# One Strassen level (seven quarter products) for the first product of the second layer

## What is computed

```python
h = x @ w_in            # x: 1536 tokens x 512, w_in: 512 x 2048
r = np.maximum(h, 0.0)
g = r * r
return g @ w_out        # w_out: 2048 x 512
```

## Time and profile before

| what | us |
|---|---|
| median of 3 runs | 483.92 (483.80 to 483.97) |
| span of the profiled execution, first to last instruction | 481.6 |
| around the span (median less span) | 2.3 |
| TensorE busy in the span | 471.1 |
| VectorE busy | 278.1 |
| ScalarE busy | 212.9 |
| GpSimd busy | 103.8 |

### The profile page before, as it was taken

The page is one execution under the profiler, slowest core; times in us unless marked ns, Lnnn a source line. Parts: engine busy times, 40 slices in busy tenths (PEclk is TensorE's granted clock), DMA queues, the critical chain, the costliest instruction groups (busy, mean ns, idle before and its releaser), DMA issues.

```text
span 481.6 us, 7337 instructions
## 1 busy us (share of the span) xinstructions
PE 471.1 (98%) x2634; PEld 382.5 (79%) x2634; DVE 278.1 (58%) x514; ACT 212.9 (44%) x559; POOL 103.8 (22%) x155
## 2 busy tenths in 40 slices
PE   7889999999999999999999999999999999999997
PEld 5667787887788888878888888888888888888885
DVE  3899889898989888767755354322222233222232
ACT  3677777656777666242324253222222232222221
POOL 2366323231321232739930000000000000000000
PEclk9999999999999999999999999999999999999999
DMA  7931437765569424498400000200000020000002
GB/s 214 315 92 50 136 85 215 205 192 159 149 180 219 113 57 120 119 252 240 90 1 0 1 0 1 87 0 0 0 0 0 0 87 1 0 0 1 0 1 87
DMA packets 51990, 41.80 MB, mean 87 GB/s; under 512 B 28088, under 2 KB 38072, under 8 KB 51448
## 3 DMA queue, kind: packets, MB, share of 16 engines
q1 hardware_dynamic: 51192, 40.74, 29.9%
q10 hardware_dynamic: 768, 0.66, 0.5%
HBM read 30.38 MB, written 11.01 MB: 86 GB/s over the span
## 4 chain that ended last, share of the span: by engine, by line
PE 91%; DVE 3%; POOL 2%; ACT 1%; DMA 1%; issue 1%; ACTq 0%; DVEq 0%; POOLq 0%
PE score_ps L1675 27%; PE h_ps L1689 14%; PE w_ps L1516 13%; PE h_ps L1476 12%; PE w_ps L1689 7%; PE wt_ps L1689 7%; PE o_ps L1438 4%; PE score_ps L1404 2%; PE wt_ps L1404 2%; PE wt_ps L1415 1%; DMA x2T<-qT 1%; PE o_ps L1459 1%; POOL pT_own L576 1%; PE w_ps L1541 1%; DVE prob L1095 1%
## 5 line engine op out<-in xcount | busy, mean ns | idle before, releaser
L1675 PE MATMUL score_ps<-x2T_hi,w2in_hi 128*128 (+1 forms) x192 | 74.8, 389 | 0.0
L1675 PE MATMUL score_ps<-x2T_hi,w2in_lo 128*128 (+1 forms) x192 | 74.7, 389 | 0.0
L1675 PE MATMUL score_ps<-x2T_lo,w2in_hi 128*128 (+1 forms) x192 | 74.7, 389 | 0.0
L1328 DVE TENSOR_TENSOR e<-e 128x512 f32<-128x512 f32 x24 | 17.9, 744 | 82.0 <-ACT e L968 82.0
L1328 DVE TENSOR_TENSOR sq<-relu 128x512 f32<-128x512 f32 x24 | 17.2, 717 | 77.0 <-ACT relu L968 77.0
L968 ACT ACTIVATE relu<-score_ps 128x512 f32<-128x512 f32 x24 | 14.3, 597 | 90.5 <-PE score_ps L1675 90.5
L968 ACT ACTIVATE e<-score_ps 128x512 f32<-128x512 f32 x24 | 14.4, 599 | 89.7 <-PE score_ps L1675 89.7
L1675 PEld LDWEIGHTS score_ps<-x2T_lo,w2in_hi 128*128 128x128 f32 x192 | 36.0, 188 | 7.5
L1675 PEld LDWEIGHTS score_ps<-x2T_hi,w2in_hi 128*128 128x128 f32 x192 | 36.1, 188 | 7.5
L1675 PEld LDWEIGHTS score_ps<-x2T_hi,w2in_lo 128*128 128x128 f32 x192 | 36.0, 188 | 7.4
L742 ACT ACTIVATE prob<-sm,nbias 128x132 f32<-128x132 f32 (+1 forms) x96 | 37.6, 393 | 4.1 <-DVE nbias L1019 3.4
(11 more groups left out here) (192 smaller groups left out, 1095.0 us busy)
## 6 DMA issues: line engine op xcount, KB each, us to landing
u_dram<-uT SPq DMA_DIRECT2D x18, 256.0 KB, 3.2
lnT_raw<-u_dram SPq DMA_DIRECT2D x36, 128.0 KB, 2.9
w2in<-w_in SPq DMA_DIRECT2D x4, 1024.0 KB, 5.3
w2out<-w_out SPq DMA_DIRECT2D x8, 512.0 KB, 9.9
V<-v SPq DMA_DIRECT2D x12, 256.0 KB, 3.2
x2T<-x_dram SPq DMA_DIRECT2D x12, 256.0 KB, 4.8
x_dram<-x SPq DMA_DIRECT2D x44, 64.0 KB, 2.2
k_raw<-kT SPq DMA_DIRECT2D x20, 132.0 KB, 2.9
```

Of the source, the lines that this page charges most:

```text
L1328: nc.vector.tensor_tensor(sq[f % 2], relu[f % 2], relu[f % 2], ALU.mult).then_inc(sq_ready, 1)
L1675: done = mm(h2_ps[f % 2], ws[:, c, fs], xs[:, c, bass.ts(blk, BLK)], start=(c == 0 and i == 0), stop=(c == MC - 1 and i == 2))
```

## The change

The first product of layer two is done as one Strassen level (the form with seven products and fifteen sums). x (512 features x 768 tokens) and a piece of `w_in` (512 features x 2 x 128 units) are each cut in 2 x 2 quarters; four sums of quarters are made on each side, seven products of quarters are taken, and their sums are the four tiles of h. The tokens go in two passes of 768, each with 8 steps of 256 hidden units (two groups of 128): 16 steps. Token halves are 384 wide, so a product is 2 chunks x 3 = 6 matmuls of 384 columns.

Per step, each pass anew: SP loads a piece of `w_in` (two DMAs of 256 KB in rows of 512 bytes) and of `w_out` (512 KB); GpSimd makes the four sums of weights (128x256 each) and the lo parts (128x512, 128x1024, 128x256); ScalarE rounds; VectorE makes five sums with one operand in PSUM (128x384), the gate (relu times itself) and its lo parts in three parts (384, 768, 384 wide) and the lo part of `w_out` (128x1024). The x combinations (seven, 128x768 each) of pass 0 are summed by GpSimd and split by VectorE and GpSimd; those of pass 1 by VectorE in steps 2 to 6.

The relevant constants and the TensorE order:

```diff
-BLK = BANK
+PASSES = 2
+TS = T // PASSES
+TH = TS // 2
+NJ = C2 // 2
+NI = PASSES * NJ
+PRODUCTS = ((A11, B11, 0, True), (S2, T2, 1, True), (A12, B21, 0, False), (S3, T3, 1, False),
+            (S1, T1, 0, True), (A22, T4, 1, False), (S4, B22, 0, False))
+UNITS = tuple((tile, r, q) for tile, r, qs in ((0, 0, (0, 1, 2)), (1, 1, (0, 1, 2)), (2, 1, (3, 4, 5)), (3, 0, (3, 4, 5)))
+              for q in qs)
...
+            def multiply(i, n):
+                wk, xk, bank, opens = PRODUCTS[n]
...
+                if n == 0 and i:
+                    pe.wait_ge(added, 5 * i)
+                elif n == 1 and i:
+                    pe.wait_ge(added, 5 * i - 1)
+                elif n == 2:
+                    pe.wait_ge(p1_copied, i + 1)
+                elif n == 3:
+                    pe.wait_ge(added, 5 * i + 1)
+                elif n == 4:
+                    pe.wait_ge(corner_ready, i + 1)
+                elif n == 5:
+                    pe.wait_ge(added, 5 * i + 2)
+                elif n == 6:
+                    pe.wait_ge(added, 5 * i + 3)
+                for c in range(2):
+                    for k in range(3):
+                        ws, xs = ((w2_hi, xc_hi), (w2_hi, xc_lo), (w2_lo, xc_hi))[k]
+                        done = mm(prod_ps[bank], ws[i % 2][:, wk, c, :], xs[s][xk][:, c, :], start=(opens and c == 0 and k == 0),
+                                  stop=(c == 1 and k == 2), skip_group_check=True)
...
+            multiply(0, 0)
+            multiply(0, 1)
             project(NT - 2, 0, 24)
-            hidden2(0, 1, 2, 3)
+            multiply(0, 2)
+            multiply(0, 3)
             transpose_ln(NT - 1)
-            hidden2(0, 1, 3, 4)
-            project(NT - 1, 0, 12).then_inc(wo_half_read, 1)
+            multiply(0, 4)
+            project(NT - 1, 0, 12)
+            multiply(0, 5)
             project(NT - 1, 12, 24)
-            with pe.Fori(0, NB - 1) as blk:
-                block_b(blk, True)
-            block_b(NB - 1, False)
+            multiply(0, 6)
+            for i in range(1, NI):
+                multiply(i, 0)
+                multiply(i, 1)
+                project2(i - 1, 0, 4)
+                multiply(i, 2)
+                multiply(i, 3)
+                project2(i - 1, 4, 8)
+                multiply(i, 4)
+                multiply(i, 5)
+                multiply(i, 6)
+                project2(i - 1, 8, 12)
+            project2(NI - 1, 0, 12)
```

`added` counts VectorE's sums, five a step: sum_2, sum_3, lower_right, lower_left, upper_right. VectorE's order in a step:

```diff
+            for i in range(1, NI):
+                sum_2(i)
+                split_g(i - 1, 2)
+                if i == NJ + 1:
+                    copy_y(0, (3, 5))
+                split_wy(i)
+                sum_3(i)
+                gate_corner(i)
+                lower_right(i)
+                split_g(i, 0)
+                lower_left(i)
+                gate_sum(i, 1)
+                if i == 2:
+                    sum_x(T1, 0, x_quarter(0, 1), x_quarter(0, 0))
+                    sum_x(T2, 1, x_quarter(1, 1), x_combination(1, T1))
+                elif i == 3:
+                    sum_x(T3, 2, x_quarter(1, 1), x_quarter(0, 1))
+                    split_x(1, B11)
+                elif i == 4:
+                    split_x(1, T2)
+                    split_x(1, B21)
+                elif i == 5:
+                    split_x(1, T3)
+                    split_x(1, T1)
+                    dve.wait_ge(xc_split[T2], 2)
+                    sum_x(T4, 3, x_quarter(1, 0), x_combination(1, T2))
+                elif i == 6:
+                    split_x(1, T4)
+                    split_x(1, B22)
+                elif i == NJ:
+                    copy_y(0, (1,))
+                upper_right(i)
+                split_g(i, 1)
+                gate_sum(i, 2)
```

GpSimd's list:

```diff
+                if t == NT - 3:
+                    sum_x(T1, 0, x_quarter(0, 1), x_quarter(0, 0))
+                    sum_x(T2, 1, x_quarter(1, 1), x_combination(0, T1))
+                    sum_x(T3, 1, x_quarter(1, 1), x_quarter(0, 1))
                 if t + 2 < NT and not alone(t + 2):
                     gather_sinks(t + 2)
...
-            for f in range(C2):
-                if f == 3:
-                    inverse_std(NT - 1)
-                    pool.wait_ge(ln_ready, 2 * NT)
-                fs = slice(f * P, (f + 1) * P)
...
+            pool.wait_ge(scored, PAIRS * NT)
+            sum_w2(0)
+            split_w2_first(0)
+            split_w2_sums(0)
+            split_w2_last(0)
+            split_x(B21)
+            split_x(T3)
+            inverse_std(NT - 1)
+            pool.wait_ge(xc_split[T2], 1)
+            sum_x(T4, 3, x_quarter(1, 0), x_combination(0, T2))
+            for i in range(1, NI):
+                sum_w2(i)
+                split_w2_first(i)
+                split_w2_sums(i)
+                split_w2_last(i)
```

ScalarE's list in a step:

```diff
+            for i in range(1, NI):
+                copy_p1(i)
+                round_g(i - 1, 2)
...
+                round_wy(i)
+                if i + 1 < NI:
+                    round_w2(i + 1)
+                corner(i)
+                round_g(i, 0)
+                if i + 1 < NI:
+                    round_w2_sums(i + 1)
...
+                round_g(i, 1)
```

In layer one two orders change. TensorE's last step does 8 of the 24 products of tile 9 ahead of hidden(11), and 16 behind it:

```diff
-                project(n - 2, 0, 24)
+                project(n - 2, 0, 8)
                 pe.wait_ge(u_ready, 2 * n)
                 hidden(n, 0, 24)
+                project(n - 2, 8, 24)
```

```diff
             square_x2(NT - 4)
             for part in range(len(LN_PARTS)):
                 split_lnT(NT - 3, part)
+            split_xT(NT - 1)
             normalize_hidden(NT - 2)
-            split_xT(NT - 1)
             square_u(NT - 2)
-            split_x2T(0)
-            square_x2(NT - 3)
+            split_x(0, B11)
+            split_x(0, T2)
             hidden_max(NT - 1, 0)
             hidden_max(NT - 1, 1)
             hidden_max_all(NT - 1)
...
+            sum_2(0)
+            square_x2(NT - 3)
             normalize_hidden(NT - 1)
+            split_x(0, T1)
+            split_x(0, T4)
+            split_x(0, B22)
             square_x2(NT - 2)
...
+            sum_3(0)
             for part in range(len(LN_PARTS)):
                 split_lnT(NT - 1, part)
```

More of the change, by code:

```diff
@@ L513, in _ @@
[L513 to L525, removed]
@@ L529, in side_loads @@
+            for i in range(2, NI):
+                load_wy(i)
+                if i + 1 < NI:
+                    load_w2(i + 1)
+                if i == NJ + 2:
+                    store_y(0)
+            store_y(1)
+            sp.wait_ge(y_stored, 16 * (PASSES * YT + 1))
         def side_loads(act):
@@ L956, in _, with copy_y @@
+            def copy_y(s, qs):
+                for q in qs:
+                    act.wait_ge(y_done, YT * s + q + 1)
+                    nc.scalar.copy(y[:, q, :], y_ps[q]).then_inc(y_copied_act, 1)
             for part in range(len(LN_PARTS)):
@@ L1368, in _ @@
+            split_g(NI - 1, 2)
+            copy_y(1, (1, 3, 5))
         @block.tensor
@@ L1660, in _ @@
             last_step()
-            def hidden2(blk, f, first=0, last=MC):
-                g = blk * C2 + f
-                if first == 0:
-                    pe.wait_ge(w2in_split, f + 1)
-                    if f == 0:
-                        pe.wait_ge(x2T_split, blk + 1)
-                    if f >= 2 or since(blk, 1):
-                        pe.wait_ge(relu_ready, g - 1)
-                fs = slice(f * P, (f + 1) * P)
-                for c in range(first, last):
-                    for i in range(3):
-                        ws, xs = ((w2in_hi, x2T_hi), (w2in_hi, x2T_lo), (w2in_lo, x2T_hi))[i]
-                        done = mm(h2_ps[f % 2], ws[:, c, fs], xs[:, c, bass.ts(blk, BLK)],
-                                  start=(c == 0 and i == 0), stop=(c == MC - 1 and i == 2))
-                if last == MC:
-                    done.then_inc(h2_done, 1)
@@ new lines, in project2 @@
+            def project2(i, first, last):
+                j, s = i % NJ, i // NJ
+                for n in range(first, last):
+                    tile, r, q = UNITS[n]
+                    if n == 0:
+                        pe.wait_ge(wy_split, i + 1)
+                    if n % QH3 == 0:
+                        pe.wait_ge(g_split, 3 * i + (1, 2, 2, 3)[tile])
+                    if i == 0 and n == 2 * QH3:
+                        pe.wait_ge(x2_squared, NT)
+                    if s and j == 0 and r == q // QH3:
+                        pe.wait_ge((y_copied_act, y_copied_dve)[q % 2], q // 2 + 1)
+                    rows = slice(q % QH3 * P, (q % QH3 + 1) * P)
+                    for k in range(3):
+                        gs, ws = ((g_hi, wy_hi), (g_hi, wy_lo), (g_lo, wy_hi))[k]
+                        done = mm(y_ps[q], gs[i % 2][:, tile, rows], ws[i % 2][:, r, :],
+                                  start=(j == 0 and r == q // QH3 and k == 0), stop=(j == NJ - 1 and r != q // QH3 and k == 2))
+                    if j == NJ - 1 and r != q // QH3:
+                        done.then_inc(y_done, 1)
```

(2 more changed lines are left out.)

466 lines of the change are left out of this document (291 added, 175 removed).

## The result

| what | before | after |
|---|---|---|
| median, us | 483.86 (482.77 to 483.97, 4 runs) | 496.51 (495.46 to 497.01, 4 runs) |
| ratio after/before, 95% interval | | 1.0265 (1.0247 to 1.0282) |
| profiled span | 481.6 | 494.4 |

Slower by 12.65 us; the forecast was 492.8, in a range of 473 to 497.

What follows compares the result with a forecast made beforehand. The prediction took the kernel to be bound by the columns TensorE streams. From 483.9 us it took off 14.1 for products and added 4.8 (hidden(10)), 5.1 (seam) and 13.1 (x pieces): 492.8 us, range 473 to 497.

Steps and rivals of the forecast that it cites:

- products: Layer two's first product: 672 matmuls of 384 columns at 0.173 us replace 576 of 512, saving 14.1 us.
- hidden(10) late: Layer one: GpSimd's three x sums take turns with VectorE's normalizing and x split, delaying hidden(10) by 4.8 us.
- seam, waits: Where the layers meet: waits before project(10), project(11) and step 1's first product, +5.1 us, bounds 0.5 and 5.5.
- x pieces, steps 2 to 6: VectorE's x pieces, ahead of upper_right, take turns with GpSimd's weight sums and delay the next step's first product: +13.1 us.
- rival 4: Layer two's first product: weight load surfaces at 384 columns, 0.214 us each, 27 us more, near 520; chance 0.03.
- A steady step: New loop, step without x pieces: 15.44 us; more than 15.5 us would show the prediction wrong.
- P6's cover of 0.2 us: Each step's last of seven products: the lower_right sum is ready at 11.45 us, product due at 11.67, so no wait.
- rival 3: The 0.2 us cover of each step's seventh product fails too, 0.3 us in 15 steps: 497.3 us; chance 0.1.
- the second product keeps 576 matmuls of 512 columns: Layer two's second product: matmul number and width unchanged, priced at the old 0.227 us each, so no change in time.
- Each microsecond in which it waits is lost: TensorE throughout: bound by columns streamed, so a wait was priced at its own length, with no clock cost added.
- 1 and 2: First: all covers hold, 471.9 us, chance 0.2. Second: only the x pieces are free, 481.3 us, chance 0.14.
- rival 1: Covers hold: GpSimd's instructions fall between VectorE's; x sums, seam and x pieces cost bare time: 471.9 us; chance 0.2.

Runs made afterwards that it cites:

- upper_first: Kernel after, with VectorE in steps 2 to 6 doing upper_right, split_g and the last gate_sum before the x pieces: 484.58 us, ratio 1.0017.
- filled_wait: Kernel after, with 15 matmuls of no use put into TensorE's wait before hidden(10): 493.15 us, ratio 1.0198.
- ln_first: Kernel after, with VectorE doing tile 10's square, sum_3(0) and tile 11's split before the T4 and B22 splits: 493.41 us, ratio 1.0181.
- three_orders: Kernel after, with x pieces behind upper_right, GpSimd's x sums behind tile 10's x split, tile 11's split before T4 and B22's: 476.04 us, ratio 0.9838.

## Why the prediction was right, and what it had wrong

The sign held, and so did the place and the cause ("GpSimd and VectorE taking turns at one port") of each loss that was forecast. Two costs of another kind were not in the sum. The terms, in us, predicted and as the trace of after shows them:

| term | predicted | measured | from |
|---|---|---|---|
| products | -14.1 | -13.7 | 0.1733 apart, but 0.175 in P2 to P6 of even steps |
| hidden(10) late | +4.8 | +4.3 | 20.58 against 16.24 from hidden(9) |
| slow clock behind it | 0 | +2.9 | 8.33 against 5.44 |
| seam, waits | +5.1 | +3.5 | 0.4 + 2.4 + 1.0, less 0.3 there before |
| slow clock behind it | 0 | +1.6 | 4.26 + 1.39 against 2.99 + 1.06 |
| x pieces, steps 2 to 6 | +13.1 | +11.1 | 10.6 of waits less step 1's 0.7, and 5 x 0.24 |
| slow clock behind step 5 | 0 | +1.3 | 3.49 against 2.16 |
| pace of the second product | 0 | +2.6 | 2.79 and 2.75 for 12 against 2.72 |
| sum | +8.9 | +13.6 | spans: 494.4 - 481.6 = +12.8, and 0.8 that the trace of after was ahead |

The 0.24 is what a wait costs beside its length at full clock: the listed idle time begins with a matmul's result, 0.16 us after its slot, and the 12 matmuls behind a wait take some 0.08 more.

- **Products.** Right: 384 columns come every 0.1733 us, the columns and the same 0.0133, but for the 0.4 us of the even steps. The weight load did not surface (rival 4).
- **A steady step.** Said 15.44, measured 15.6 to 15.8. By the prediction's own sign ("if a step without pieces takes more than 15.5 us") this part is wrong. P6's cover of 0.2 us held in all 15 steps, so rival 3 (497.3) falls, though its total lies nearest. The step that failed is "the second product keeps 576 matmuls of 512 columns", taken at the old price: it kept the number and not the pace.
- **Steps 2 to 6.** "In turns" is what the timeline shows, instruction by instruction. The forecast's P0 at 17.7 us into the step came at 17.5 to 17.6, and 19.3 with three pieces at 19.0. The term is smaller than 13.1 for this and because the steady step was longer to begin with. `upper_first` shows the price: 11.9 us, waits and clock together, with its own new 0.5 taken off.
- **hidden(10).** GpSimd's sums took 1.88 and 1.98 us, said 1.85; the wait ended 1.2 us earlier than I had it, of which 0.8 is the start of the trace.
- **The seam.** project(11) waited 2.13, said 3.0, P0 of step 1 0.74, said 0.75. project(10) had 1.7 and took 0.4: the chain behind hidden_exp was drawn too late. That term was oversized.
- **The step that is missing.** "Each microsecond in which it waits is lost" was too kind: in the trace of after a wait of 3.57, of 2.13 and of 3.05 us was each followed by matmuls at half pace, 5.8 us in all. I read "the granted clock is full in every slice" as a fact about the kernel and not as one about its gaps: before, TensorE's longest was the 1.7 us at the start of the kernel, and every later one at most 0.93. `filled_wait` shows it for hidden(10), where the wait is filled, and `ln_first`, where the seam's wait is gone, fits it. But the 1.6 and 1.3 us are not owed to the length of a wait alone, since the profiled run of filled_wait had the same two waits at full clock. What decides there stays open. The Trainium skill, TensorE: Matmul & The Clock Gate, Part 1, says that the engine's clock is throttled by default and released by activity; the traces agree for hidden(10), with spacings of 0.427 us behind the empty wait and 0.227 us behind the filled one for the same matmul.
- **The rivals of the other sign.** 1 and 2 wanted VectorE and GpSimd out of each other's way. They are not: an x piece takes 1.5 us beside GpSimd in after. The Trainium skill, SBUF — State Buffer, in Terms and in Who interferes with whom, calls the shared port pair an exclusive lock held for the whole instruction, and says that a VectorE instruction with two SBUF inputs contends with a GpSimd one that reads SBUF. The trace agrees, and adds that both engines alternate when both have work queued. Part of the gain of rival 1 (471.9) is to be had all the same, by order: three_orders, with the same sums and splits at the port as after, is at 476.0.

Three waits were put too high, by 0.5 + 1.6 + 2.0 = 4.1 us together, and what was missing comes to 5.8 + 2.6 + 0.4 = 8.8. That these set each other off in part is luck: the total was 3.7 us too low, and 496.5 lies within the range, half a microsecond from its end.

## What to carry to other kernels

When a change gives two engines that share a port more to do, list for each result that the bound engine waits for what stands ahead of it in the other engines' lists, and move everything else behind it: here 20 us lay in three such places, and no operation had to be made cheaper. On a TensorE that never waits, a new wait can cost more than its length. Give it a range: here the upper end was 2.9, 1.6 and 1.3 us of matmuls at half clock behind waits of 3.57, 2.13 and 3.05 us, and the lower end nothing, as one run had it behind the last two. A smaller product is only worth its columns if its sums are off the other engines' critical order.

## What was not expected of the hardware

- The granted clock fell after waits of 2.13, 3.05 and 3.57 us (0.66 to 0.83 in stretches of ten us), from 2.4 to 1.2 GHz by the spacing, and did not after four waits of about 1.7 us. In the profiled run of filled_wait it did not fall after waits of 2.13 and 3.06 us either. Fifteen matmuls without a use in the wait before hidden(10) went with a clock of 1.00 behind it, 2.8 us less for hidden(10), and a kernel 3.4 us faster.
- A 512-column matmul of the second product came 0.2325 us after the one before it in odd steps and 0.2283 to 0.2300 in even ones, at a granted clock of 1.00, against 0.2267 before. The alternation does not follow the buffers of its weights, and the slow pace is there with DMA and all other engines still; it ends 24 matmuls before the end. Of the 384-column ones those of P2 to P6 alternate the other way, 0.1733 in odd steps and 0.1750 in even ones.
